# Three edits to the opening of an attention and two-expert kernel: order of SyncE's loads, order of own-token products, one matrix product less

## What is computed

```python
for t in range(S):
    cur = einsum('bhd,bhe->bhde', u * kt, vt)                 # the token's own term
    y[:, :, t] = einsum('bhd,bhde->bhe', rt, state + cur)
    state = wt[..., None] * state + einsum('bhd,bhe->bhde', kt, vt)
x = y as [3072 tokens, 384]
h = x @ w_in1;  h = h * softmax(h);  h = layernorm(h) * g_ln;  x = h @ w_out1     # 1024 wide
g = maximum(0.01 * (x @ w_in2), x @ w_in2);  out = g @ w_out2                     # 2048 wide
```

## Time and profile before

| | |
|---|---|
| median of three executions | 785.93 us (785.57 to 787.09) |
| the profiled execution | 786.64 us, of which the span from the first to the last instruction is 784.8 us |
| PE busy | 777.4 us, 99% of the span |
| DVE, ACT, POOL busy | 520.1, 341.5, 174.5 us |
| moved by DMA | 45.89 MB, mean 58 GB/s over the span |

### The profile page before, as it was taken

The page is one execution under the profiler, slowest core; times in us unless marked ns, Lnnn a source line. Parts: engine busy times, 40 slices in busy tenths (PEclk is TensorE's granted clock), DMA queues, the critical chain, the costliest instruction groups (busy, mean ns, idle before and its releaser), DMA issues.

```text
span 784.8 us, 12142 instructions
## 1 busy us (share of the span) xinstructions
PE 777.4 (99%) x4638; PEld 734.1 (94%) x4638; DVE 520.1 (66%) x1024; ACT 341.5 (44%) x676; POOL 174.5 (22%) x199
## 2 busy tenths in 40 slices
PE   8999999999999999999999999999999999999998
PEld 4789999899999999999999999999999999999998
DVE  7998999966665676657747567485674766543432
ACT  3577654434344354343434443344343444334333
POOL 4632422321222211212212123022120221100000
PEclk9999999999999999999999999999999999999999
DMA  9961022212113022030120210202202111000001
GB/s 277 278 234 41 26 66 66 57 41 66 36 31 96 1 66 60 7 95 13 54 66 1 97 49 18 66 9 88 66 1 66 36 62 31 1 1 30 1 1 35
DMA packets 20065, 45.89 MB, mean 58 GB/s; under 512 B 1968, under 2 KB 14768, under 8 KB 20000
## 3 DMA queue, kind: packets, MB, share of 16 engines
q1 hardware_dynamic: 15952, 37.17, 15.7%
q10 hardware_dynamic: 4048, 7.87, 3.0%
HBM read 40.31 MB, written 4.72 MB: 57 GB/s over the span
## 4 chain that ended last, share of the span: by engine, by line
PE 80%; DVE 1%; issue 0%; ACT 0%; DVEq 0%
PE BANKS L1186 56%; PE MISC L1186 20%; PE BANKS L1365 2%; PE MISC L1210 1%; PE MISC L1203 1%; DVE ki L870 0%; DVE W2L L1018 0%; DVE att L860 0%; DVE A L883 0%; DVE Rraw L1002 0%; DVE RL L1009 0%; DVE X2L L1024 0%; ACT X2H L739 0%; ACT OUT L745 0%; DVE diag L890 0%
## 5 line engine op out<-in xcount | busy, mean ns | idle before, releaser
L1186 PE MATMUL BANKS<-RH,W4H 128*128 128x384 f32 x384 | 135.4, 353 | 0.0
L1186 PE MATMUL BANKS<-X2H,W3H 128*128 128x384 f32 x384 | 130.8, 341 | 0.2 <-DVE X2L L1024 0.2
L1186 PE MATMUL BANKS<-X2L,W3H 128*128 128x384 f32 x384 | 129.3, 337 | 0.0
L1186 PE MATMUL BANKS<-X2H,W3L 128*128 128x384 f32 x384 | 129.2, 336 | 0.0
L1186 PE MATMUL BANKS<-RH,W4L 128*128 128x384 f32 x384 | 129.1, 336 | 0.0
L1186 PE MATMUL BANKS<-RL,W4H 128*128 128x384 f32 x384 | 129.0, 336 | 0.0
L1002 DVE TENSOR_TENSOR Rraw<-BANKS,Rraw 128x384 f32<-128x384 f32 x128 | 70.6, 552 | 87.1 <-ACT Rraw L718 86.1
L718 ACT ACTIVATE Rraw<-BANKS 128x384 f32<-128x384 f32 x128 | 62.6, 489 | 137.2 <-PE BANKS L1186 136.9
L722 ACT ACTIVATE RH<-Rraw 128x384 fp32r<-128x384 f32 x128 | 67.1, 524 | 100.8 <-DVE Rraw L1002 100.8
L870 DVE RECIPROCAL ki<-att 112x128 f32<-112x128 f32 x96 | 89.5, 937 | 0.0
L1009 DVE TENSOR_TENSOR RL<-Rraw,RH 128x384 fp32r<-128x384 f32 x128 | 71.6, 560 | 22.5 <-ACT RH L722 22.5
(11 more groups left out here) (141 smaller groups left out, 1495.7 us busy)
## 6 DMA issues: line engine op xcount, KB each, us to landing
att<-rkw SPq DMA_DIRECT2D x23, 672.0 KB, 4.8
rtok<-r_tok SPq DMA_DIRECT2D x22, 192.0 KB, 2.5
ktok<-k_tok SPq DMA_DIRECT2D x22, 192.0 KB, 2.9
vtok<-v_tok SPq DMA_DIRECT2D x22, 192.0 KB, 3.6
out<-OUT SPq DMA_DIRECT2D x7, 576.0 KB, 4.3
W3raw<-w_in ACTq DMA_DIRECT2D x2, 1536.0 KB, 10.4
W4raw<-w_out ACTq DMA_DIRECT2D x1, 3072.0 KB, 16.6
W1raw<-w_in SPq DMA_DIRECT2D x2, 768.0 KB, 12.3
```

Of the source, the lines that this page charges most:

```text
L1186: return nc.tensor.matmul(dst, lhsT, rhs, start=start, stop=stop, skip_group_check=True)
```

## The change

SP's list gets another order and two waits. The decays of chunk 1 become a transfer of their own with a semaphore of their own, issued behind chunk 0's channels-first parts; then u and chunk 0's tokens follow. Then SP waits until r and k of chunk 0 have landed, issues r and k of chunk 1, waits until u has landed, and issues the first half of W1 and the rest as before. POOL's `decayed_queries` and DVE's `undecayed_keys` get a wait for the load of their chunk in the first three chunks. On POOL, own-token part 0 of chunk 0 goes ahead of the end keys. On DVE, the own sums go ahead of reciprocal 0 of chunk 1. On PE, the `unread(1)` behind the state product of chunk 0 goes.

```diff
+        ld_decay = [sem("ld_decay0"), sem("ld_decay1")]
 SyncE
+            def load_decay(m):
+                sp.dma_start(att[:, m, 2, :, :]..., rkw[m * PD:(m + 1) * PD, 2 * PAIRS * CH:3 * PAIRS * CH]).then_inc(ld_decay[m], 16)
...
-                if first(b, m) and m == 0:
-                    sp.dma_start(to[:, 2, :, :]..., rkw[0:PD, 2 * PAIRS * CH:3 * PAIRS * CH]).then_inc(ld_decay, 16)
+                if first(b, m) and m < 2:
+                    if m == 0:
+                        load_decay(0)
                     both, part = slice(0, 2), slice(0, 2 * PAIRS * CH)
...
             load_T(0, 0)
+            load_decay(1)
+            sp.dma_start(ub[:, :], u.partition_broadcast(CH)).then_inc(ld_u, 16)
+            load_tok(0, 0)
+            sp.wait_ge(ld_T[0], 16)
             load_T(0, 1)
-            load_tok(0, 0)
-            sp.dma_start(ub[:, :], u.partition_broadcast(CH)).then_inc(ld_u, 16)
+            sp.wait_ge(ld_u, 16)
             columns = w_in1.rearrange("(k p) n -> p k n", p=128)
             sp.dma_start(w1[:, :, 0:512], columns[:, :, 0:512]).then_inc(ld_w1a, 16)
 GpSimd
             def decayed_queries(b, m):
+                if first(b, m):
+                    wait_T(pool, b, m)
...
             decayed_queries(0, 0)
-            end_keys(0, 0)
             pool.wait_ge(ld_u, 16)
             own_token(0, 0, 0)
+            end_keys(0, 0)
             own_token(0, 0, 1)
 VectorE
-                if first(b, m) and m == 0:
-                    dve.wait_ge(ld_decay, 16)
+                if first(b, m) and m < 2:
+                    dve.wait_ge(ld_decay[m], 16)
...
             def undecayed_keys(b, m, portion=(0, PAIRS)):
+                if first(b, m):
+                    wait_T(dve, b, m)
...
-            inverse(0, 1, 0)
             own_sums(0, 0)
-            inverse(0, 1, 1)
+            for a in (0, 1):
+                inverse(0, 1, a)
             take_y(0, 0)
 TensorE
             first_state(0)
-            unread(1)
             first_transposes(0)
```

More of the change, by code:

```diff
@@ L257, in build @@
         consts, chain = sem("consts"), sem("chain")
-        ld_decay, ld_w1a, filled = sem("ld_decay"), sem("ld_w1a"), sem("filled")
+        ld_decay = [sem("ld_decay0"), sem("ld_decay1")]
+        ld_w1a, filled = sem("ld_w1a"), sem("filled")
         ld_w3a = sem("ld_w3a")
@@ L396, in _ @@
         def _(sp):
+            def load_decay(m):
+                sp.dma_start(att[:, m, 2, :, :].rearrange("p a t -> p (a t)"),
+                             rkw[m * PD:(m + 1) * PD, 2 * PAIRS * CH:3 * PAIRS * CH]).then_inc(ld_decay[m], 16)
             def load_T(b, m):
@@ L409, in load_T @@
                 both, part = slice(0, 3), slice(0, 3 * PAIRS * CH)
-                if first(b, m) and m == 0:
-                    sp.dma_start(to[:, 2, :, :].rearrange("p a t -> p (a t)"),
-                                 rkw[0:PD, 2 * PAIRS * CH:3 * PAIRS * CH]).then_inc(ld_decay, 16)
+                if first(b, m) and m < 2:
+                    if m == 0:
+                        load_decay(0)
                     both, part = slice(0, 2), slice(0, 2 * PAIRS * CH)
```

## The result

The changed kernel takes 789.13 us in the median of 20 executions (785.97 to 794.69), the kernel before 786.75 (785.57 to 788.33) beside it. The ratio is 1.0031, 95% interval 1.0018 to 1.0044: **slower by 0.3%**, where 0.2% faster was forecast. The spread is as telling as the median: 2.8 us before, 8.7 after. Nine of the 20 executions kept a mean granted clock of 0.999 or more and have a median of 786.5 us; the other eleven have 0.993 to 0.998 and a median of 790.4. A mean of 0.995 over 788 us is about 8 us at 1.2 instead of 2.4 GHz (half a per cent of 788 us, twice, since the clock is halved there). So two things need an explanation: why undisturbed executions gain nothing that can be told, and why more than half lose clock.

A forecast was written before the change was run, and what follows sets the result against it. PE was taken to bound the kernel (777.4 of 784.8 us busy), its earlier start to shorten it. Expert products 1.70 us earlier, less 0.1 at the mask, gave 1.6 us: 785.93 to 784.3 us, range 783.5 to 786.3.

The forecast's parts named there:

- Scans of chunk 1: On DVE, the scans no longer wait for chunk 1's load and start at about 9.77, 0.28 us earlier.
- Own sums: On DVE, the own sums start at 12.22, behind the masks, with r*u*k there since 11.4.
- rival B: W1's first half lands late, at 18.7; PE starts 0.95 us later than before, about 787.6 us in all; chance 5%.
- Landing of the tokens: In the new load order u and chunk 0's tokens land at 9.3 us, between 9.2 and a slow-rate 10.3.
- Take y: DVE's step that PE's transposes of y wait for comes at 14.34 instead of 16.04, 1.70 us earlier.
- that is covered, by 0.25 us: POOL's delayed end keys end at 12.5, ahead of PE's transposes that want them at 12.75.
- rival A: Tokens land at 10.3, PE's transposes come 0.85 us later; gain only 0.75 us, 785.2 us; chance 16%.
- Mask of chunk 1: DVE's first mask ends at 21.54, PE wants it at 21.75; cover just used up, 0.1 us lost.
- rival C: TensorE's clock falls ahead of the expert products, without wide products there; 3.3 us cost, 787.6 us; chance 8%.
- What else is queued behind the SP waits: Chunk 2, tokens of chunk 1 and W1's second half come in the same order with the same bytes ahead.
- rival D: The gain is lost behind 20 us to an engine without room, giving 784.8 to 785.9 us; chance 10%.
- fixed cost of a completion: By the skill's rule SP's waits bring W1 up to 2 us later, sum about 1 us worse; queued bytes hide it.

## Why the prediction was wrong, point by point

- **PE bounds, and its start sets the end**: right. In every profiled execution with the full clock and without a later wait PE's lead at 20 us is there at 60 us within 0.1 us. Up to its last product it drifts by up to 0.4 us more, and what lies behind that differs by 0.8 us between executions, so a gain of some tenths can't be read off one time.
- **Scans of chunk 1**: 9.77 forecast, 9.74 measured. **Own sums**: 12.22 and 12.19. The wait for W1 (rival B) never came up: X released the expert products.
- **Landing of the tokens, mis-sized**: 9.3 taken, 9.9 in the profile, 9.8 to 11.0 in the eight profiled executions of the same order, and 11.3 in the one without waits. My slow bound of 10.3 came from one execution and was no bound.
- **Take y**: 14.34 forecast, 14.71 measured, from 0.38 us of PE waiting for the end keys. Expert 1 16.46 instead of 16.08. The step "that is covered, by 0.25 us" failed; I had named the price of the cover as lateness alone (rival A, 0.85 us at 10.3).
- **Mask of chunk 1**: 0.1 us put, 0.27 measured (the lead goes from 1.32 to 1.05 us at 22.40).
- **The step that failed most** is the price of that cover: own-token products ahead of the end keys were taken to cost nothing, or 0.85 us where the tokens are late, and rival A and rival C stood as two cases with 16% and 8%. They are one: late tokens make PE stand still ahead of the transposes, and the fall follows. That edit alone, in the kernel before, gave 1.0035, and 11 of the 20 executions of the changed kernel lost clock. C's price was about right, 3.3 us forecast and 3.9 measured (790.4 against 786.5 between the two kinds of execution), and so was its sign. Its reading of PE's first products as the low level holds as well: 0.80 us a record there, 0.82 at a granted clock of 0.50 (4.92 us for six). But I tied it to the unread product, which alone does nothing. And the row I set against it had no idle time in it; I said so, but looked only at the 0.6 us ahead of the expert products, and that wait for X (0.58 us) is in the profiles with the full clock too. The idle time that mattered lies ahead of the end-key transposes, where I had put none. The Trainium skill's sentence on transposes ("TensorE: Matmul & The Clock Gate", Part 4) told nothing here; with the gap filled the same seven transposes ran at the full clock.
- **What else is queued behind the SP waits**: "comes in the same order with the same bytes ahead" was put without a look at where each load is first used. Chunk 3 landed 0.3 us ahead of its use before (37.1 and 37.37), beside two loads of 1.5 MB on ACT's queue that the change brings forward by 1.1 and 1.3 us (to 18.57 and 21.45). It landed at 39.7, DVE waited 2.74 us, PE 1.0. Before it the tokens of chunk 2 were late as well (1.93 us on POOL, 0.35 on PE). The sum has no term for it; rival D (gain lost behind 20 us) had 10% and the wrong cause.
- **The Trainium skill's fixed cost of a completion** ("DMA: Bandwidth & Descriptors", "Anatomy of one DMA"): the first half of W1 landed at 15.9 with the waits, 16.3 without them and 15.5 in the kernel before, and without them neither bytes nor tokens came sooner (227 GB/s, tokens at 11.3). So in these runs the waits didn't cost what that rule gives. The section gives its figure for transfers that GpSimd issues, and these are SyncE's; the 3.1 us that I called the same size are half as much again.
- **The base**: 1.70 us counted from a u at 12.37, where other executions of that order had 11.1 to 11.65. Of the forecast gain 0.7 to 1.05 us (17.78 against 17.07 and 16.73) was the luck of one profile.
- **The range** ended at 786.3, below the kernel before's own median of 786.75 in 20 executions; three executions had given 785.93.

What stays open: why the DMA engines move fewer bytes in some executions, how often chunk 3 is late outside profiled executions, why executions of the changed kernel with the full clock still reach from 786.0 to 789.1 us, and how large the unread product's part in the rarer short falls (0.997 and 0.998, none of them in a profiled execution) is. A semaphore of its own for v, so that POOL's first products wait for r and k alone, wasn't tried. No variant beat the kernel before.

## What to carry to other kernels

Before an engine's step is moved ahead of another, ask who waits for the one pushed back, and take the landing it will now hang on from several executions, not from one: a cover of 0.25 us under a load that varies by over 1 us is no cover. Don't price a stall of TensorE between small products at its own length alone: here a stall of over 1 us cost some 4 us with the fall of the clock behind it. And when a list of loads is reordered, note for each load, on every queue, how long it lands ahead of its first use, since the smallest of these margins goes first.

## What the runs showed of the hardware

- A pause of 1.25 to 1.81 us of TensorE, between small products, was followed by 7 to 10 us at the granted clock of 0.50 in all four profiled executions that had it; a pause of 0.38 us at the same place was not, nor were pauses of 0.75 us somewhat later, ahead of the transposes of y, in two others. With two unread products in the pause the clock stayed at 0.999 or more in 11 of 11 executions.
- The landing of the same load in the same order differs by over 1 us from one execution to the next (u between 11.1 and 12.3 us in the five profiled executions of the old order), while the durations of DVE's and POOL's instructions in the rows shown mostly repeat to 0.02 us.
